# A 64-column weight slice for one of five down-projection matmuls in a convolution and two-MLP kernel

## What is computed

```python
x = conv7(x, softmax(weight))                       # 16384 x 192
h = np.maximum(x @ w_in1, 0.0);  x = (h * h) @ w_out1
h = x @ w_in2
g = np.where(h > 0, h, np.exp(np.minimum(h, 0)) - 1)
out = g @ w_out2
```

## Time and profile before

| | |
|---|---|
| median of the runs | 2363.64 us |
| runs | 2362.62, 2363.64, 2364.51 us |
| profiled execution, span from first to last instruction | 2362.3 us |
| TensorE busy | 2328.2 us, 10240 matmuls |
| weight loads | 1925.1 us, 10240 loads |
| VectorE, ScalarE, GpSimd busy | 1693.1, 1520.5, 57.0 us |
| mean granted TensorE clock | 0.998 |

### The profile page before, as it was taken

The page is one execution under the profiler, slowest core; times in us unless marked ns, Lnnn a source line. Parts: engine busy times, 40 slices in busy tenths (PEclk is TensorE's granted clock), DMA queues, the critical chain, the costliest instruction groups (busy, mean ns, idle before and its releaser), DMA issues.

```text
span 2362.3 us, 33660 instructions
## 1 busy us (share of the span) xinstructions
PE 2328.2 (99%) x10240; PEld 1925.1 (81%) x10240; DVE 1693.1 (72%) x2807; ACT 1520.5 (64%) x2766; POOL 57.0 (2%) x48
## 2 busy tenths in 40 slices
PE   5999999999999999999999999999999999999999
PEld 3888888888888888888888888888888888888887
DVE  7767777677776677776777767776667777677777
ACT  4766666666666666666666666666666666666664
POOL 6200000000000000000000000000000000000000
PEclk9999999999999999999999999999999999999999
DMA  4000000000000000000000000000000000000000
GB/s 143 19 8 16 9 16 16 9 14 14 12 16 16 7 16 9 16 16 7 16 9 16 16 16 7 16 9 16 16 7 16 9 16 16 7 16 14 12 7 14
DMA packets 66477, 38.19 MB, mean 16 GB/s; under 512 B 1952, under 2 KB 64416, under 8 KB 66464
## 3 DMA queue, kind: packets, MB, share of 16 engines
q1 hardware_dynamic: 66464, 38.03, 5.6%
HBM read 25.44 MB, written 12.58 MB: 16 GB/s over the span
## 4 chain that ended last, share of the span: by engine, by line
PE 97%; DVE 1%; DMA 0%; issue 0%; ACT 0%; SPq 0%; DVEq 0%
PE bank_a L286 10%; PE bank_b L287 10%; PE bank_a L283 10%; PE bank_a L282 10%; PE bank_b L284 10%; PE bank_h L265 10%; PE bank_h L263 10%; PE bank_h L266 10%; PE bank_h L264 10%; PE bank_h L262 10%; DVE conv_b L448 0%; DVE conv_a L448 0%; DVE act_lo L487 0%; DMA raw_down<-in_moe_w_out_dram 0%; DMA x_cols<-in_x_dram 0%
## 5 line engine op out<-in xcount | busy, mean ns | idle before, releaser
L487 DVE TENSOR_TENSOR act_lo<-act,act_hi 128x512 fp32r<-128x512 f32 x1024 | 712.7, 696 | 451.6 <-ACT act L353 448.7
L358 ACT ACTIVATE expo<-bank_h 128x512 f32<-128x512 f32 x512 | 306.5, 599 | 509.6 <-PE bank_h L266 506.3
L342 ACT ACTIVATE relu<-bank_h 128x512 f32<-128x512 f32 x512 | 306.4, 598 | 278.8 <-PE bank_h L266 273.5
L262 PE MATMUL bank_h<-mov_hi_a,up_hi_a 128*128 128x512 f32 x1024 | 399.1, 390 | 20.2 <-DVE mov_lo_b L453 20.2
L286 PE MATMUL bank_a<-act_lo,down 128*128 128x512 f32 x1024 | 399.5, 390 | 9.1 <-DVE act_lo L487 9.0
L263 PE MATMUL bank_h<-mov_lo_a,up_hi_a 128*128 128x512 f32 x1024 | 399.3, 390 | 0.0
L264 PE MATMUL bank_h<-mov_hi_a,up_lo_a 128*128 128x512 f32 x1024 | 399.1, 390 | 0.0
L266 PE MATMUL bank_h<-mov_lo_b,up_b 128*128 128x512 f32 x1024 | 399.1, 390 | 0.0
L265 PE MATMUL bank_h<-mov_hi_b,up_b 128*128 128x512 f32 x1024 | 399.1, 390 | 0.0
L284 PE MATMUL bank_b<-act_hi,down 128*128 128x512 f32 x1024 | 398.8, 389 | 0.0
L282 PE MATMUL bank_a<-act_hi,down 128*128 128x512 f32 x1024 | 398.8, 389 | 0.0
(11 more groups left out here) (45 smaller groups left out, 1861.0 us busy)
## 6 DMA issues: line engine op xcount, KB each, us to landing
x_cols<-in_x_dram SPq DMA_DIRECT2D x32, 536.0 KB, 4.3
out_dram<-res_a SPq DMA_DIRECT2D x32, 256.0 KB, 2.6
raw_up<-in_moe_w_in_dram SPq DMA_DIRECT2D x8, 512.0 KB, 6.3
out_dram<-out_b SPq DMA_DIRECT2D x32, 128.0 KB, 2.3
raw_down<-in_moe_w_out_dram SPq DMA_DIRECT2D x8, 384.0 KB, 7.0
x_cols<-in_x_dram SPq DMA_DIRECT2D x1, 512.0 KB, 4.1
taps<-in_weight_dram SPq DMA_DIRECT2D x1, 7.0 KB, 1.7
```

The costliest lines, as they stand in the source:

```text
L262: pe.matmul(bank, hi, hi_a, start=True, stop=False)
L487: dve.tensor_tensor(act_lo[s][:, :], act32[s][:, :], act_hi[s][:, :].bitcast(F32), ALU.subtract)\
```

## The change

In every step, the matmul of `act_lo` for the last 64 output features takes only the 64 columns of high weight parts, and writes only partitions 0 to 63 of `bank_b`. The low by low products are no longer added for these features. In the last step of each half (`last`, 64 of the 1024 steps) the full matmul with `act_hi` is moved from before the wait for `lo_ready` to the end of the step. There it ends the accumulation for all 128 partitions and raises `down_done`. The number of matmuls stays the same.

```diff
                 pe.wait_ge(hi_ready, g + 1)
                 pe.matmul(a, w[:, HI_A], act_hi[s][:, :], start=first, stop=False)
                 pe.matmul(a, w[:, LO_A], act_hi[s][:, :], start=False, stop=False)
-                pe.matmul(bb, w[:, HI_LO_B], act_hi[s][:, :], start=first, stop=False)
+                if not last:
+                    pe.matmul(bb, w[:, HI_LO_B], act_hi[s][:, :], start=first, stop=False)
                 pe.wait_ge(lo_ready, g + 1)
                 pe.matmul(a, w[:, HI_A], act_lo[s][:, :], start=False, stop=last)
-                pe.matmul(bb, w[:, HI_LO_B], act_lo[s][:, :], start=False, stop=last).then_inc(down_done, 1)
+                done = pe.matmul(bank_b[h][0:DB, :], w[:, P:D], act_lo[s][:, :], start=False, stop=False)
+                if last:
+                    done = pe.matmul(bb, w[:, HI_LO_B], act_hi[s][:, :], start=False, stop=True)
+                done.then_inc(down_done, 1)
```

## The result

The changed kernel takes 2383.91 us (median of four runs, 2383.18 to 2384.95), the kernel before, in the same series, 2363.97 us (2362.62 to 2364.51). The ratio is 1.0086, with a 95% interval of 1.0074 to 1.0098. So the change made it slower by 19.9 us, and the forecast of no change was wrong. The profiled execution of the changed kernel took 2384.52 us, with a span of 2382.6 us.

The account below looks back on a forecast made before the run. The prediction took TensorE as the bound, 10240 matmuls at a fixed 226.6 ns each plus some 30 us of start and 5 of end. All terms were zero, giving 2363.6 us against the median, range 2349.5 to 2366.5.

Parts of the forecast that it names:

- The matmul with 64 output columns: Price of the 1024 narrower matmuls: taken as zero, because the 512 moving columns set the cost.
- 13.3 ns rest: Per matmul, the measured 226.6 ns less 213.3 for 512 moving columns at 2.4 GHz; taken as independent of weight columns.
- Rival A: Switching width around line 287 exposes a load each way, 0.11 us each: 225 us slower, 2589 us; chance 0.15.
- Rival B: In the matmul spacing, a narrower load shrinks the 13.3 ns: 6.8 to 13.6 us faster, 2356.8 to 2350.0; chance 0.22.
- C: The machine loads or drains 128 columns anyway: time of no change, shown by the load's record; within no change's 0.63.
- The order in the last steps: In 64 last steps line 286 wants act_lo 0.227 us sooner; slack covers it, so zero.
- The sum: All parts of the change over the whole span added up: 0 us on 2362.3 us.
- the start: Before the steady stream of matmuls, some 30 us of start beyond the matmuls' fixed cost.

Follow-up runs that it names:

- e13: The changed kernel with 97 weight columns in the low matmul instead of 64; 2362.82 us.
- e7: The kernel before, all weights 128 columns wide, but the low matmul for the last 64 output columns moves 480 tokens instead of 512; 2398.35 us.
- e8: The kernel before, 128 weight columns everywhere, but the low matmul for the last 64 output columns takes only rows 0 to 63; 2768.41 us.
- e11: The changed kernel with 100 weight columns in the low matmul instead of 64; 2364.00 us.
- e6: Eight of ten matmuls take 64 columns, except the down-projection's in the first and last step of a half, leaving out products the changed kernel takes; 2393.70 us.
- e16: The kernel before, 128 weight columns everywhere, but the low matmul for the last 64 output columns moves 256 tokens instead of 512; 2276.45 us.
- e1: The changed kernel with the low matmul 128 columns wide again, keeping only its order in each half's last step; 2364.21 us.

## Why the prediction was wrong

**The step that failed** is "The matmul with 64 output columns": "I take zero". It is the one price that the trace of before didn't have. I had bounded it from -13.6 to +225 us, and the 20 us lie inside that. Then I chose by an argument about the 13.3 ns rest, which told only whether narrower weights could give something back. It said nothing of whether they could take something. Measured are 20.0 ns for each narrow matmul, in the distances behind it.

**The spacing was a rhythm, not a price.** The 226.7 ns are what TensorE does in an undisturbed stream. Once disturbed, it goes through other distances, most of them 228 to 236 ns, before it finds them again. This stood in the trace of before, in the lines that follow:

```profile
30.67 0.40 PE L287 MATMUL bank_b<-act_lo,down 128*128 128x512 f32 x1
30.91 0.39 PE L262 MATMUL bank_h<-mov_hi_a,up_hi_a 128*128 128x512 f32 x1
31.13 0.40 PE L263 MATMUL bank_h<-mov_lo_a,up_hi_a 128*128 128x512 f32 x1
31.36 0.39 PE L264 MATMUL bank_h<-mov_hi_a,up_lo_a 128*128 128x512 f32 x1
31.60 0.39 PE L265 MATMUL bank_h<-mov_hi_b,up_b 128*128 128x512 f32 x1
31.82 0.39 PE L266 MATMUL bank_h<-mov_lo_b,up_b 128*128 128x512 f32 x1
```

The distances, from the start times, are 236, 228, 232, 231 and 227 ns, together 21 ns more than five of 226.7. The changed kernel pays much the same in each of 1024 steps. I read only the first 0.34 us of that restart and not the five distances behind it.

That the two agree so well is in part luck, since other restarts of the same trace cost other amounts. Here is the one with the shortest recovery:

```profile
47.83 0.50 PE L286 MATMUL bank_a<-act_lo,down 128*128 128x512 f32 x1 [1.58 <-DVE act_lo L487]
48.17 0.40 PE L287 MATMUL bank_b<-act_lo,down 128*128 128x512 f32 x1
48.40 0.39 PE L262 MATMUL bank_h<-mov_hi_a,up_hi_a 128*128 128x512 f32 x1
48.63 0.39 PE L263 MATMUL bank_h<-mov_lo_a,up_hi_a 128*128 128x512 f32 x1
48.86 0.39 PE L264 MATMUL bank_h<-mov_hi_a,up_lo_a 128*128 128x512 f32 x1
```

After the 0.33 us come 233 and 231 ns and then the old spacing, 11 ns in all. The restarts at 35.22 and 51.69 us cost 30 and 25 ns, and one of e13, at 60.40 us, costs nothing. What they share is the way back. The longest course without a break is that of e13 from 25.99 us on: 237, 233, 236, 224, 231, 236, 228, 233, 231 and then 226.7 ns, and the shorter ones end, give or take a ns or two, in its last distances. The nine distances of e7 are that whole course, those of the changed kernel its last four. So a disturbance seems to cost by how far back it throws TensorE on this course; what decides that isn't shown.

**Rival A** (slower, chance 0.15) had the right side and the right part: going from 128 columns to 64 and back disturbs TensorE, with nothing to hide it. Its size was wrong. It priced an exposed load per switch, 225 us. Measured are 20.0 ns x 1024 = 20.5 us, and no load is exposed. Its prices had a hole between 0 and 113 us, and the result fell into it. The exposed load exists, and costs even more than I had put, when the rows are halved (e8).

**Rival B** (faster) is refuted by e11 and e13, with loads 24 and 26 ns shorter at the old spacing, and in e6 eight narrow loads of ten made the step longer. Its room, the 13.3 ns, isn't a fixed cost of each matmul either, as I had argued. In e16 the matmul with half the moving columns has half of it: 113.3 ns against 106.7 for 256 columns at 2.4 GHz. There it went with the moving columns; in the disturbed stream of e7 the matmul of 480 has 13.3 ns again, so a strict proportion isn't shown.

**What held.** The number of matmuls and the granted clock stayed. The load stayed hidden and its record became shorter, so C is out. It fell by some 27 ns for each 32 columns (188, 161, 134, 108 ns for 128, 96, 64, 32). The Trainium skill's rule ("TensorE: Matmul & The Clock Gate", section on LDWEIGHTS), columns divided by 1.2 GHz, gives 26.7 for 32 columns. The traces agree with that slope, and each record is some 81 ns longer than the rule gives for it. The order in the last steps cost nothing (e1), and waits for `act_lo` stayed at 9.1 us. The sum failed in one term. One reading was off without effect: the start isn't some 30 us over the matmuls' price but 36 (75 us less 171 x 0.2266), since the earlier trace rows has a granted clock of 0.95 there and not only waits; both kernels have the same start.

**What stays open.** The runs show the trigger and the course, not the cause. Loading the weights, the array itself, or the writing of PSUM may react to an unused group. Each narrow matmul has a narrow load of its own and writes fewer partitions of PSUM, so the runs don't part the three. Nor is it shown whether 64 columns select another tiling mode, which the prediction had asked: no record shows the mode, and if they do, it exposes no load here. Open is also why three groups cost more than two or one. All narrow slices left the upper columns unused; one that leaves out the lower ones wasn't tried. A stream with narrow matmuls throughout was not tried, since e6 keeps one or more full ones in each step.

## What to carry to other kernels

Where TensorE is busy without a gap and the loads are hidden, as here, fewer weight columns brought nothing at any width. A lone float32r matmul of 96 columns or fewer among full ones costs 20 to 35 ns here, and one that uses half of the rows costs 400 ns. So fill the unused columns with anything that does no harm (97 columns are as good as 128). If a steady spacing is measured, look also at the first matmuls after several waits. Here they were 0 to 30 ns off in all, and an irregular matmul in every step, where it cost anything, cost 20 to 35 ns with few weight columns and, with fewer moving columns, 27 and 47 ns against the 113 and 13 that it saved itself (e16 and e7). That gives the size of such a risk before a change is tried, but not the exact price.

## What the runs showed that I had not expected

- 97 columns cost nothing and 96 cost 34.7 ns per step, with loads of 162 and 161 ns.
- The order of prices isn't that of the widths: 96 (34.7 ns) and 90 (33.4) are dearer than 64, 50 and 32 (20.0 each).
- 32 moving columns fewer in one matmul of ten made the step 33.4 ns longer, 256 fewer made it 86.6 ns shorter.
- A matmul of 64 rows among matmuls of 128 rows costs twenty times as much as one of 64 columns: 400 ns against 20.
